# Spreading the softmax reciprocals of an attention kernel: two DMAs through DRAM per head in place of transposes and PSUM copies

## What is computed

```python
scores = scale * np.matmul(q, k.transpose(0, 1, 3, 2))
scores = np.where(mask, scores, -1000000000.0)
scores = scores - np.max(scores, axis=-1, keepdims=True)
attn = np.exp(scores)
attn = attn / (np.sum(attn, axis=-1, keepdims=True) + 1e-09)
return np.matmul(attn, v).astype(np.float32)
```

## Time and profile before

| what | value |
|---|---|
| three runs | 814.16, 816.96, 819.42 us, median 816.96 |
| the profiled execution's own time | 818.39 us |
| its span on the chip | 816.5 us |
| PE busy | 778.7 us, 95% of the span |
| DVE busy | 481.5 us, 59% |
| ACT busy | 383.7 us, 47% |
| POOL busy | 232.4 us, 28% |
| 16 DMA engines | 17.9% of their time |

### The profile page before, as it was taken

The page is one execution under the profiler, slowest core; times in us unless marked ns, Lnnn a source line. Parts: engine busy times, 40 slices in busy tenths (PEclk is TensorE's granted clock), DMA queues, the critical chain, the costliest instruction groups (busy, mean ns, idle before and its releaser), DMA issues.

```text
span 816.5 us, 11692 instructions
## 1 busy us (share of the span) xinstructions
PE 778.7 (95%) x3776; PEld 632.6 (77%) x3776; DVE 481.5 (59%) x838; ACT 383.7 (47%) x718; POOL 232.4 (28%) x150
## 2 busy tenths in 40 slices
PE   3999999999989879999999999999999999999998
PEld 2787778777777768888888888888887888888886
DVE  4899999999989961156665656656576211210220
ACT  2788889888889963344231232323143211211221
POOL 3345555545565454563220211202022000000000
PEclk9999999999999999999999999999999999999999
DMA  5342223232242122233110101101010000001001
GB/s 147 75 97 62 64 61 80 79 81 63 61 119 71 44 78 65 90 103 104 52 51 1 52 0 51 51 1 51 1 53 0 1 26 26 1 14 39 0 0 51
DMA packets 14095, 42.17 MB, mean 52 GB/s; under 512 B 2386, under 2 KB 4434, under 8 KB 14066
## 3 DMA queue, kind: packets, MB, share of 16 engines
q1 hardware_dynamic: 14066, 41.79, 17.9%
HBM read 34.61 MB, written 3.15 MB: 46 GB/s over the span
## 4 chain that ended last, share of the span: by engine, by line
PE 73%; DVE 11%; issue 7%; ACT 5%; DMA 1%; DVEq 0%; SPq 0%; POOL 0%; ACTq 0%
PE psum L984 53%; PE psum L1071 8%; DVE top L728 4%; PE psum L910 3%; PE psum L923 3%; DVE pt_lo L742 3%; ACT prob L501 2%; PE psum L899 2%; PE psum L893 2%; ACT pt_hi L524 1%; DVE x_lo L846 1%; DVE exp_at L735 1%; DMA stage<-in_w_out 1%; PE psum L884 1%; DVE qm L721 1%
## 5 line engine op out<-in xcount | busy, mean ns | idle before, releaser
L501 ACT ACTIVATE prob<-psum,exp_at 128x768 f32<-128x768 f32 x96 | 96.5, 1005 | 29.8 <-DVE exp_at L735 29.8
L742 DVE TENSOR_TENSOR pt_lo<-psum,pt_hi 128x384 fp32r<-128x384 f32 x192 | 98.1, 552 | 11.1 <-ACT pt_hi L524 9.6
L728 DVE TENSOR_REDUCE top<-psum 128x1 f32<-128x768 f32 x96 | 91.0, 948 | 4.3 <-PE psum L899 4.0
L618 ACT ACTIVATE relu<-psum 128x512 f32<-128x512 f32 x48 | 28.6, 597 | 137.3 <-PE psum L984 137.3
L910 PE MATMUL psum<-ident,prob 128*128 128x128 f32 x576 | 85.1, 281 | 7.3 <-DVE pt_lo L742 6.9
L984 PE MATMUL psum<-x_hi,w_c 128*128 128x512 f32 (+1 forms) x288 | 90.6, 396 | 0.0
L984 PE MATMUL psum<-x_hi,w_b 128*128 128x512 f32 (+1 forms) x288 | 90.6, 396 | 0.0
L524 ACT ACTIVATE pt_hi<-psum 128x384 fp32r<-128x384 f32 x192 | 84.2, 495 | 11.0 <-PE psum L910 10.1
L869 DVE TENSOR_TENSOR ab<-psum,a_sb 128x512 f32<-128x512 f32 x24 | 16.6, 692 | 121.3 <-ACT a_sb L668 121.3
L823 DVE SCALAR_TENSOR_TENSOR relu<-psum,relu 128x512 f32<-128x512 f32 x48 | 33.1, 690 | 87.8 <-ACT relu L618 82.7
L910 PEld LDWEIGHTS psum<-ident,prob 128*128 128x128 f32 x576 | 65.4, 141 | 22.1 <-DVE pt_lo L742 13.2
(11 more groups left out here) (92 smaller groups left out, 1516.7 us busy)
## 6 DMA issues: line engine op xcount, KB each, us to landing
raw<-in_qk SPq DMA_DIRECT2D x30, 384.0 KB, 5.0
stage<-in_w_out SPq DMA_DIRECT2D x12, 512.0 KB, 3.4
stage<-in_w3t SPq DMA_DIRECT2D x8, 512.0 KB, 3.2
stage<-in_w_in SPq DMA_DIRECT2D x8, 512.0 KB, 3.3
stage<-in_w SPq DMA_DIRECT2D x8, 512.0 KB, 3.2
raw_v<-in_v SPq DMA_DIRECT2D x16, 192.0 KB, 2.6
qm<-both_hi SPq DMA_DIRECT2D x16, 192.0 KB, 2.7
out<-out_sb SPq DMA_DIRECT2D x12, 256.0 KB, 2.0
```

Of the source, the lines that this page charges most:

```text
L501: act.activation(prob[:, t % 3], score[t % 2], ACT.Exp, bias=exp_at[:, t % 2, 1:2], scale=exp_at[:, t % 2, 0:1], accum_out=rsum[:, (t // 3 ...
L728: dve.tensor_reduce(top[:, t % 2, 1:2], score[t % 2], AX.X, ALU.max, negate=True).then_inc(top_done, 1)
L742: dve.tensor_tensor(pt_lo[at], turned[part].rearrange("p (j q) -> p j q", j=3), pt_hi[at].bitcast(F32), ALU.subtract).then_inc(pt_lo_done, 1)
```

## The change

The reciprocals are now taken once a head, for its six tiles together, by DVE at t % 6 == 4. SP writes them to a DRAM buffer `r_rows` of 16 x 768 floats (`sums_out`) and reads the head's row back, repeated over 64 partitions, straight into `r_sb` (`sums_in`). `inverse_rows` on PE and `r_copy` on ACT are gone, and with them `rrow_done` and `r_copied`; `dots` waits for `bits_done` alone. `r_sb` is now one row of 768 per partition, with one half of the partitions for each head of a pair. `x_of` waits for the arrival of the second DMA. `o_add` waits for x_done of two units further back. In SP's program `sums_out` stands ahead of `load_qk` and `sums_in` behind it; in the last pairs they stand among the loads of weights. SP's loop over pairs is written out, and DVE's loop starts at the third pair.

```diff
+            def sums_out(h, par, pr):
+                sp.wait_ge(rinv_done, h + 1)
+                sp.dma_start(r_rows[bass.ds(h, 1)].rearrange("o (j p) -> p (o j)", p=P),
+                             rinv[:, par], allow_slow_non_contiguous=True).then_inc(r_out[par], 16)
+
+            def sums_in(h, par, pr):
+                sp.wait_ge(r_out[par], 16 * (pr + 1))
+                after(sp, x_done, 2 * h - 2)
+                sp.dma_start(r_sb[HALVES[par]],
+                             r_rows[bass.ds(h, 1)].broadcast_to([HD, SEQ])).then_inc(r_in[par], 16)
...
                         copy_q_hi(h + 2, k)
                         load_v(h + 2, k)
+                    if last and k == 1:
+                        load_w(W3 + 1, 1, w3t[1])
+                    sums_out(h, k, pr)
+                    if not last:
                         load_qk(h + 4, k)
+                    elif k == 0:
+                        load_w(W3, 0, w3t[0])
+                    sums_in(h, k, pr)
...
-            def x_of(u, unit):
+            def x_of(u, unit, pr):
                 pool.wait_ge(o_sum_done, u + 1)
-                pool.wait_ge(r_copied, u + 1)
+                pool.wait_ge(r_in[unit // 2], 16 * (pr + 1))
...
-            def r_copy(u, unit):
-                act.wait_ge(rrow_done, u + 1)
-                after(act, x_done, u - 3)
-                rows = slice(0, HD) if unit < 2 else slice(HD, P)
-                act.activation(r_sb[rows, unit % 2], m_ps[rows], ACT.Copy).then_inc(r_copied, 1)
...
-                    if t % 3 == 1:
-                        row_sums(n + 1, u, t // 3)
+                    if t % 6 == 4:
+                        row_sums(n + 1, h, k)
...
-                    if t % 3 == 1:
-                        inverse_sums(u, t // 3)
+                    if t % 6 == 4:
+                        inverse_sums(h, k, pr)
...
-            def inverse_rows(u, unit):
-                pe.wait_ge(rinv_done, u + 1)
-                for j in range(3):
-                    tr = pe.transpose(m_ps[:, j * P:(j + 1) * P],
-                                      rinv[:, unit % 2, j:j + 1].broadcast_to([P, P]), ident[:, :])
-                tr.then_inc(rrow_done, 1)
...
-                            after(pe, r_copied, 2 * h)
+                            pe.wait_ge(bits_done, 2 * h + 2)
...
-                    if t % 3 == 2:
-                        if t % 6 == 2 and not (last and k == 1):
-                            pe.wait_ge(bits_done, 2 * h + 4)
-                        else:
-                            pe.wait_ge(r_copied, u)
-                        inverse_rows(u, t // 3)
...
-                after(dve, x_done, u - 1)
+                after(dve, x_done, u - 3)
```

More of the change, by code:

```diff
@@ L69, in attention_mlp @@
             vs = sb("vs", [P, 2, TILES, 2 * HD], FR, a)
-            r_sb = sb("r_sb", [P, 2, HALF], F32, a)
+            r_sb = sb("r_sb", [P, SEQ], F32, a)
             o_part = sb("o_part", [P, HALF], F32, a)
@@ L82, in attention_mlp @@
             exp_at = sb("exp_at", [P, 2, 2], F32, a)
-            rsum = sb("rsum", [P, 2, 3], F32, a)
-            rsum_e = sb("rsum_e", [P, 2, 3], F32, a)
-            rinv = sb("rinv", [P, 2, 3], F32, a)
+            rsum = sb("rsum", [P, 2, TILES], F32, a)
+            rsum_e = sb("rsum_e", [P, 2, TILES], F32, a)
+            rinv = sb("rinv", [P, 2, TILES], F32, a)
         w_c = sb("w_c", [P, 4 * WCH], FR)
@@ L136, in attention_mlp @@
         m_ps = psum[:, 7, 0:HALF]
+        r_rows = nc.dram_tensor("r_rows", [HEADS, SEQ], F32)
         qk_in = [sem("qk_in0"), sem("qk_in1")]
@@ L168, in attention_mlp @@
         rinv_done = sem("rinv_done")
-        rrow_done = sem("rrow_done")
-        r_copied = sem("r_copied")
+        r_out = [sem("r_out0"), sem("r_out1")]
+        r_in = [sem("r_in0"), sem("r_in1")]
         o_part_done = sem("o_part_done")
@@ L270, in _ @@
             pair(0)
-            with sp.Fori(1, PAIRS - 2) as pr:
+            for pr in range(1, PAIRS - 2):
                 pair(pr)
@@ L279, in _ @@
                 load_v(h + 2, k)
+                sums_out(h, k, PAIRS - 2)
                 load_w(2 + k, k, w_out2[:, (2 + k) * WCH:(3 + k) * WCH])
+                sums_in(h, k, PAIRS - 2)
             pair(PAIRS - 1, last=True)
-            for k in range(2):
-                load_w(W3 + k, k, w3t[k])
             with sp.Fori(1, FT // 2) as ip:
@@ L359, in v_lo @@
                                    ALU.subtract).then_inc(v_lo_done, 1)
-            def x_of(u, unit):
+            def x_of(u, unit, pr):
                 pool.wait_ge(o_sum_done, u + 1)
-                pool.wait_ge(r_copied, u + 1)
+                pool.wait_ge(r_in[unit // 2], 16 * (pr + 1))
                 rows = slice(0, HD) if unit < 2 else slice(HD, P)
                 at = slice((unit % 2) * HALF, (unit % 2 + 1) * HALF)
-                pool.tensor_tensor(x_raw[rows, at], o_sum[rows, unit % 2], r_sb[rows, unit % 2],
+                pool.tensor_tensor(x_raw[rows, at], o_sum[rows, unit % 2], r_sb[rows, at],
                                    ALU.mult).then_inc(x_done, 1)
@@ L394, in pair @@
                 if not first:
-                    x_of(4 * pr - 2, 2)
+                    x_of(4 * pr - 2, 2, pr - 1)
                     pool.wait_ge(x_done, 4 * pr - 1)
@@ L406, in pair @@
                         w_out2_low(2)
-                    x_of(4 * pr - 1, 3)
+                    x_of(4 * pr - 1, 3, pr - 1)
                     pool.wait_ge(x_done, 4 * pr)
@@ L419, in pair @@
                     pool.wait_ge(x_lo_done, pr)
-                x_of(4 * pr, 0)
+                x_of(4 * pr, 0, pr)
                 pool.wait_ge(x_done, 4 * pr + 1)
@@ L431, in pair @@
                     pool.wait_ge(q_scaled, 2 * pr + 5)
-                x_of(4 * pr + 1, 1)
+                x_of(4 * pr + 1, 1, pr)
                 pool.wait_ge(x_done, 4 * pr + 2)
@@ L448, in _ @@
             pool.wait_ge(w_lo_done, W3 + 2)
-            x_of(2 * HEADS - 2, 2)
+            x_of(2 * HEADS - 2, 2, PAIRS - 1)
             pool.wait_ge(x_done, 2 * HEADS - 1)
-            x_of(2 * HEADS - 1, 3)
+            x_of(2 * HEADS - 1, 3, PAIRS - 1)
             pool.wait_ge(x_done, 2 * HEADS)
@@ L491, in v_high, with exps @@
                 act.activation(vs[:, par, :, 0:HD], raw_v[:, par], ACT.Copy).then_inc(v_hi_done, 1)
-            def exps(n, t, u):
+            def exps(n, t, h):
                 act.wait_ge(exp_at_done, n + 1)
                 after(act, turn_done, 2 * n - 4)
-                if t % 3 == 0:
-                    after(act, rsum_done, u - 1)
+                if t % 6 == 0:
+                    after(act, rsum_done, h - 1)
                 act.activation(prob[:, t % 3], score[t % 2], ACT.Exp, bias=exp_at[:, t % 2, 1:2],
                                scale=exp_at[:, t % 2, 0:1],
-                               accum_out=rsum[:, (t // 3) % 2, t % 3:t % 3 + 1]).then_inc(exp_done, 1)
+                               accum_out=rsum[:, (t // 6) % 2, t % 6:t % 6 + 1]).then_inc(exp_done, 1)
             def o_copy(u, unit):
@@ L559, in pair @@
                     if not (last and t > 9):
-                        exps(n + 2, (t + 2) % 12, 4 * pr + (t + 2) // 3)
-                    if t % 3 == 2:
-                        r_copy(4 * pr + t // 3, t // 3)
+                        exps(n + 2, (t + 2) % 12, 2 * pr + (t + 2) // 6)
                     if t % 6 in (3, 4) and not last:
@@ L743, in pt_low, with row_sums, inverse_sums @@
                                   pt_hi[at].bitcast(F32), ALU.subtract).then_inc(pt_lo_done, 1)
-            def row_sums(n, u, unit):
+            def row_sums(n, h, par):
                 dve.wait_ge(exp_done, n + 1)
-                dve.tensor_scalar(rsum_e[:, unit % 2, :], rsum[:, unit % 2, :], EPS, None,
+                dve.tensor_scalar(rsum_e[:, par, :], rsum[:, par, :], EPS, None,
                                   ALU.add).then_inc(rsum_done, 1)
[L751 to L755, removed]
+            def inverse_sums(h, par, pr):
+                dve.wait_ge(rsum_done, h + 1)
+                after(dve, r_out[par], 16 * pr)
+                dve.reciprocal(rinv[:, par, :], rsum_e[:, par, :]).then_inc(rinv_done, 1)
             def rows_of(unit):
@@ L790, in pair @@
                         bit_rows(h + 1, 1 - k, t % 6, pr + k)
-                    if t % 3 == 1:
-                        row_sums(n + 1, u, t // 3)
+                    if t % 6 == 4:
+                        row_sums(n + 1, h, k)
                     if ahead:
                         exp_at_of(n + 3, t + 3)
-                    if t % 3 == 1:
-                        inverse_sums(u, t // 3)
+                    if t % 6 == 4:
+                        inverse_sums(h, k, pr)
             pair(0, first=True)
-            with dve.Fori(1, PAIRS - 1) as pr:
+            pair(1)
+            with dve.Fori(2, PAIRS - 1) as pr:
                 pair(pr)
```

## The result

The changed kernel takes 927.45 us (927.32 to 929.63, five runs) against 816.91 us: a ratio of 1.136, interval 1.133 to 1.138. That is 110 us slower, far outside the range of the prediction (801 to 839). Its profiled execution has a span of 925.6 us.

The account below looks back on a forecast made before the run. The prediction took PE, DVE and ACT together, all nearly full in the attention stage, as the bound. Removed work -8, waits +2 and the end +1 gave -5 against 818.4, 813.4, or 812 us against the median; range 801 to 839.

Parts of the forecast that it names:

- The two DMAs: when do they land?: At a pair's start: sums_out lands in 4 us, sums_in's data 7.4 us behind the start, after load_qk.
- The outer bound of 10 us: Upper bound on sums_out's landing: 768 packets at the kernel's mean packet time, 8.0 + 2.0 us.
- Rival 2: At x_of's wait for r_in: slow sums_out holds POOL, then v_lo; about 840 us, at 10 us 860 and more; 22%.
- Removed work, 8 us: Attention stage: removed transposes, copies and DVE sums and reciprocals gain 8 us, bounds 4 and 13.
- conflict that moves: Small DVE instructions blocked by POOL work, as x_of moves in time: 0, plus or minus 3 us.
- Rival 3: DVE stays nearly full and moved POOL work blocks it; the 8 us shrink to 3; 817 us by the median; 11%.
- Who waits for it: Later x_of delays v_lo in first halves; PE misses 0.3 us seven times: +2 us, from 0 to 6.
- covered unless `sums_out` takes 8 us: SP's issue of copy_bits, 7.9 us behind a pair's start: not delayed, since SP is free by 3.8.
- The end: Stage end: last reciprocals pass both DMAs, PE waits 1.8 us before fused part 2; net +1 us, -1 to +4.
- m_ps: PE's dots no longer waits for r_copied; the bits_done wait replacing it was over earlier: 0.
- `o_add`: Its looser wait was never named as a releaser: 0.
- SP's written-out loop: Writing out the loop of SP, idle nearly all the time: 0.

Follow-up runs that it names:

- the store alone: Changed kernel with the scattered store issued, no sums_in, r_sb a constant and no x_of wait for it: 892.0 us.
- the run without DMAs: Changed kernel without sums_out, sums_in and the wait for r_in, r_sb set once to a constant: 819.2 us, 0.999 of the kernel before.
- the pair of runs with POOL's waits: Three POOL waits a pair for exp_at, added to the changed kernel stripped of both DMAs (801.2 us) and to the kernel before (809.9 us).
- the repaired kernels: Changed kernel storing 24-byte runs: 827.9 us; also with sums_in ahead of q and k: 826.3; also with three POOL waits a pair: 811.6.
- the packed form with `sums_in` early: Changed kernel storing 24-byte runs per partition, with sums_in ahead of the q and k loads: 826.3 us, 1.007 of the kernel before.

## Why the prediction was wrong

**The step that failed** is "The two DMAs: when do they land?", and in it the sentence "I take **4 us**". The store took 9.9. The row behind it, sb_col, bounds 4-byte packets as loads into SBUF, each to another partition; the store puts 16 of them into each 64 bytes of DRAM, and the runs above show that the step from one float to the next in DRAM alone makes the difference between 2.2 and 9.9 us. The outer bound of 10 us, from the mean packet, held the value. The 10.5 ns a packet of the Trainium skill (DMA: Bandwidth & Descriptors, Bandwidth), which I set aside by that row, gave about 10 too, as an estimate, but not for the right reason: it comes from loads issued by GpSimd, and by the packet 768 that are 64 bytes apart should have taken as long, where the trace has 2.2 us.

**Rival 2** named the right place and the right point ("a `sums_out` of about 5 us"), and it was given 22%. Its price at 10 us, "860 and more", was open upwards, and for good reason, since two of its terms were missing or too small. The first is the queue: the rival held q and k back by 2 us at a store of 7, and the bits only by SP's program, but behind a store of 10 q and k landed 6.8 us late and the bits behind them, and the store alone costs 73 us. The second is the clock: in PE's idle gaps it fell to its lower level, 0.83 in the mean of the stage. What that cost was not measured by itself; as an estimate, the changed kernel's PE is busy for 799.6 us and that of the run without DMAs, with as many instructions, for 773.9, so 26 us of work are longer, part of which may lie beside other waits.

**Removed work, 8 us.** The run without DMAs gave 0, so as a forecast of this change the term was wrong; the pair of runs with POOL's waits gives 8 to 12. The second term that failed is the "conflict that moves", put at 0 plus or minus 3: in the run without DMAs it added 13 us of exp_at, which is enough to swallow the whole gain. In the changed kernel itself exp_at takes 28.7 us, less than the 31.1 before, so there the 110 us don't come from it; it is what kept the repaired kernels from gaining. It was read from one pair of rows as a nuisance; in the timeline of before exp_at and q_lo start within 0.05 us of each other at six of their 14 meetings, which could be seen. Rival 3 described this and had 11%. The first reading was also a little off: ACT's 30.3 of 35 us is 13% from full and not within a tenth.

**Who waits for it.** With a fast store (packed, q and k ahead) r_sb landed 5.4 us from its issue, where the forecast had 4.1, and PE waited for v_lo five times, by up to 1.7 us: the predicted 0.3 a pair was of the right kind (7.8 us in all against 2). `copy_bits` "covered unless `sums_out` takes 8 us" was right as far as it went.

**The end.** Predicted: PE waits 1.8 us ahead of part 2, with a store of 4. With a store of 8 it was 7.5, since the load of r_sb, put at 2.6 like raw_v, took 5.4 as well though no load stood ahead of it; in the packed form with `sums_in` early PE waited 0.85 us. The path was right, the load's term too small in the changed kernel.

**m_ps, `o_add`, SP's written-out loop.** Put at 0, and nothing speaks against it: PE's products into m_ps wait 1.2 us for the bucket bits in the changed kernel and 2.3 before, and no row names the other two.

## What to carry to other kernels

A DMA is judged by where its bytes fall and not by their number: a few KB of single floats, packed tightly in DRAM, held a queue for 10 us here, and what suffers first is whatever stands behind them in that queue, though nobody waits for them. Write the source's runs as they are and let the reader unscramble them. And where DVE and POOL run side by side in a fixed pattern, look at which of the two starts first at each meeting before counting on any saving: taking half a microsecond of work from another engine turned such meetings round here, and three waits a pair on the engine with time to spare were worth 7.7 us on the unchanged kernel, about as much as the work removed.

## What the runs showed of the hardware

768 stores of 4 bytes to DRAM land in 9.9 us (8.3 to 11.1) when they are packed 4 bytes apart in the order of the partitions, in 8.8 when packed with one partition's six side by side, in 2.2 when each is 64 bytes from the next and in 2.3 at 256 bytes; the same 3 KB as 128 runs of 24 bytes lands in 1.4. While the slow store is under way, DMAs issued behind it on the same queue are late: q and k took 11.8 us instead of 5.0. A 128x2 operation of DVE takes 0.16 us when it starts 0.04 us ahead of a POOL operation of 1.83 us, 1.58 when it starts 0.27 behind and 1.80 when it starts 0.05 behind; it then ends with the POOL operation. A POOL product of 64x384 with one operand read at a step of 24 bytes takes 1.21 us, with a step of 4 bytes 1.01. PE's granted clock fell from 1.00 to 0.50 in a gap in which PE had been idle since 169.6 (0.53 in the mean of 173 to 174).
